# Attention to FFN in one kernel: order of the first mix, the last unit's output and the first transposes

## The reference, cut to what matters

```python
# attention, per batch b and head h (4 x 8), 576 tokens, 64 wide; w_phi: 64 x 128
def phi(x):
    proj = einsum('bhsd,df->bhsf', x, w_phi)
    proj = proj - max(abs(proj), axis=-1)
    return concatenate([exp(proj), exp(-proj)], axis=-1)
q_p, k_p = phi(q), phi(k)
kv = einsum('bhsf,bhsd->bhfd', k_p, v);  z = sum(k_p, axis=2)
x = einsum('bhsf,bhfd->bhsd', q_p, kv) / (einsum('bhsf,bhf->bhs', q_p, z) + 1e-6)
# mix over the tokens and FFN; x is now (4, 576, 512); U: 576 x 32, V: 32 x 576
u = x + transpose(transpose(x) @ U @ V)
x2 = u + relu(u @ w_ch1) @ w_ch2          # w_ch1: 512 x 2048, w_ch2: 2048 x 512
# then a mixture of 8 experts with a held choice (not touched by the change)
```

## Time and profile before

| | before |
|---|---|
| median of three runs | 935.76 us (933.89 to 935.84) |
| the profiled execution | 933.35 us, of which the span of its instructions 931.5 |
| PE busy | 898.2 us, 96% of the span |
| DVE, ACT, POOL busy | 324.1, 250.2, 147.2 us |
| mean granted clock of PE | 0.984 |

### The profile page before, as it was taken

The page is one execution under the profiler, slowest core; times in us unless marked ns, Lnnn a source line. Parts: engine busy times, 40 slices in busy tenths (PEclk is TensorE's granted clock), DMA queues, the critical chain, the costliest instruction groups (busy, mean ns, idle before and its releaser), DMA issues.

```text
span 931.5 us, 18920 instructions
## 1 busy us (share of the span) xinstructions
PE 898.2 (96%) x7112; PEld 788.9 (85%) x7113; DVE 324.1 (35%) x612; ACT 250.2 (27%) x497; POOL 147.2 (16%) x150
## 2 busy tenths in 40 slices
PE   5999999889999999999999999999999999999996
PEld 5999999679999999889988999999877777787774
DVE  4566676421221112122123323211565252332221
ACT  3566766411111111011101111111225342332221
POOL 0211122329000000000000000034332221122111
PEclk9999999979999999999999999999999999999998
DMA  5544442103000000000000000022118151311111
GB/s 130 122 129 108 124 124 73 59 24 114 1 18 18 1 0 35 0 1 34 1 1 1 35 1 12 35 93 88 46 46 304 42 217 39 116 58 34 39 34 40
DMA packets 41884, 55.84 MB, mean 60 GB/s; under 512 B 24944, under 2 KB 25072, under 8 KB 41840
## 3 DMA queue, kind: packets, MB, share of 16 engines
q1 hardware_dynamic: 38320, 44.66, 15.6%
q0 software_dynamic: 3360, 10.49, 3.5%
q10 hardware_dynamic: 160, 0.07, 0.0%
HBM read 45.76 MB, written 9.96 MB: 60 GB/s over the span
## 4 chain that ended last, share of the span: by engine, by line
PE 90%; DVE 3%; issue 3%; ACT 1%; DMA 1%; SPq 0%; ACTq 0%; DVEq 0%; POOL 0%; POOLq 0%
PE bank L1415 22%; PE bank L1417 21%; PE bank L1416 21%; PE bank L1347 7%; PE bank L1363 4%; PE bank L1320 4%; PE bank L1460 2%; PE bank L1588 2%; PE bank L1331 2%; PE bank L1478 2%; PE bank L1483 1%; PE bank L1308 1%; PE bank L1540 1%; DMA rows<-in_moe_w 1%; ACT W L831 1%
## 5 line engine op out<-in xcount | busy, mean ns | idle before, releaser
L957 DVE SCALAR_TENSOR_TENSOR hid_lo<-bank,hid_hi 128x384 fp32r<-128x384 f32 x96 | 53.6, 558 | 320.7 <-ACT hid_hi L806 320.7
L806 ACT ACTIVATE hid_hi<-bank 128x384 fp32r<-128x384 f32 x96 | 47.2, 492 | 375.8 <-PE bank L1417 375.8
L1415 PE MATMUL bank<-uT_hi,W 128*128 128x384 f32 x384 | 130.9, 341 | 1.2 <-DVE uT_lo L974 1.2
L1417 PE MATMUL bank<-uT_hi,W 128*128 128x384 f32 x384 | 130.7, 340 | 0.0
L1416 PE MATMUL bank<-uT_lo,W 128*128 128x384 f32 x384 | 130.2, 339 | 0.0
L1415 PE MATMUL bank<-W,hid_hi 128*128 128x512 f32 x288 | 117.3, 407 | 0.0
L1417 PE MATMUL bank<-W,hid_lo 128*128 128x512 f32 x288 | 115.1, 400 | 0.0
L1416 PE MATMUL bank<-W,hid_hi 128*128 128x512 f32 x288 | 114.3, 397 | 0.0
L1347 PE MATMUL bank<-vv,kp 64*128 64x65 f32 x1152 | 78.2, 284 | 3.0 <-DVE rows L931 3.0
L1415 PEld LDWEIGHTS bank<-uT_hi,W 128*128 128x128 f32 x384 | 73.5, 192 | 5.4 <-DVE uT_lo L974 1.5
L1347 PEld LDWEIGHTS bank<-vv,kp 64*128 64x128 f32 x1152 | 75.3, 202 | 3.2 <-issue 3.2
(11 more groups left out here) (229 smaller groups left out, 1305.4 us busy)
## 6 DMA issues: line engine op xcount, KB each, us to landing
rows<-in_moe_w SPq DMA_DIRECT2D x16, 1024.0 KB, 6.6
stage<-in_moe_w_ch SPq DMA_DIRECT2D x16, 512.0 KB, 4.1
qk_raw<-in_q SPq DMA_DIRECT2D x32, 144.0 KB, 2.9
qk_raw<-in_k SPq DMA_DIRECT2D x32, 144.0 KB, 3.0
vv<-in_v SPq DMA_DIRECT2D x32, 144.0 KB, 3.1
x_rows<-rows SPq DMA_DIRECT2D x6, 768.0 KB
out<-stage,oid_now POOLq DMA_INDIRECT x20, 2.8
u_pair<-in_moe_U SPq DMA_DIRECT2D x4, 72.0 KB, 4.4
```

The costliest lines, as they stand in the source:

```text
L806: act.activation(hid_hi[:, n % 2], bank[:, HB[n % 2], 0:TOK], ACT.Relu).then_inc(hid_hi_out, 1)
L957: dve.scalar_tensor_tensor(out=hid_lo[:, n % 2], in0=bank[:, HB[n % 2], 0:TOK], scalar=0.0, in1=hid_hi[:, n % 2].bitcast(F32), op0=ALU.max ...
L1415: pe.matmul(dst, lhs_hi, rhs_hi, start=start, stop=False)
L1417: return pe.matmul(dst, lhs_lo, rhs_hi, start=False, stop=stop)
```

## The change

On DVE, the first jobs stand behind steps 16 and 17 (so behind the division of unit 14), and the division of unit 15 behind the uT jobs (`first_done`). On ACT, z_hi stands in step 17 behind `exp_k`. On PE, z stays behind step 16, and the three mixes go into step 17, between `turn_q(2)` and `output(0)`. The four uT jobs of the first block take banks 2, 3, 0 and 1 and do not wait for each other; `hidden(0, 0)` waits for one part of uT before each three matmuls; the wait for the last division (`n_out`) goes from `hidden` to `output(0, 0)`; POOL waits for the last output matmuls (`n_done`) and not for the division. The two small buffers of the division leave the overlay, since they are now used while POOL writes there.

```diff
+        den = sb("den", [P, OT[0]])
+        rden = sb("rden", [P, OT[0]])
         attn = ExitStack()
...
-        den = sb("den", [P, OT[0]])
-        rden = sb("rden", [P, OT[0]])
...
-        def attention_steps(eng, step, between=lambda s: None):
+        def attention_steps(eng, step):
...
-            for s in range(UNITS, UNITS + 3):
+            for s in range(UNITS, UNITS + 2):
                 step(s, s % 2, range(s - 2, UNITS))
-                between(s)
...
+        def side_bank(job, n):
+            if job[0] == "uT" and job[1] == 0:
+                return bank[:, (2, 3, 0, 1)[job[2]]]
+            return bank[:, SIDE[n % 2]]
+
+        def is_step(s, n):
+            return isinstance(s, int) and s == n
+
+        def ffn_order(hidden, output, side, early=lambda stage: None, first_done=lambda: None):
             n = EARLY
             for job in first_jobs[EARLY:]:
                 side(job, n)
                 n += 1
+            first_done()
             hidden(0, 0)
...
-            pool.wait_ge(n_out, OUTS * UNITS)
+            pool.wait_ge(n_done, OUTS * UNITS)
...
                 if older:
                     exp_k(s - 2, par, 2)
+                    if is_step(s, UNITS + 1):
+                        side(first_jobs[0], 0)
                     exp_q(0)
...
-                for s in range(UNITS, UNITS + 3):
+                for s in range(UNITS, UNITS + 2):
                     step(s, s % 2, range(s - 3, UNITS))
-                    early_jobs(side)(s)
+                for n in range(EARLY):
+                    side(first_jobs[n], n)
...
-            ffn_order(hidden, output, side, early)
+            ffn_order(hidden, output, side, early, lambda: step(UNITS + 2, UNITS % 2, range(UNITS - 1, UNITS)))
...
                     turn_q(2)
+                    if is_step(s, UNITS + 1):
+                        for n in range(1, EARLY):
+                            side(first_jobs[n], n)
                     output(0)
                     output(1)
+                if is_step(s, UNITS):
+                    side(first_jobs[0], 0)
...
-                if f == 0:
+                if f == 0 and b > 0:
                     pe.wait_ge(side_out, jobs_before["uT", b, KC - 1])
                 if n >= 2:
                     pe.wait_ge(hid_out, n - 1)
-                else:
-                    pe.wait_ge(n_out, OUTS * UNITS)
                 for c in range(KC):
+                    if n == 0:
+                        pe.wait_ge(side_out, jobs_before["uT", 0, c])
...
                 pe.wait_ge(hid_out, n + 1)
+                if n == 0:
+                    pe.wait_ge(n_out, OUTS * UNITS)
...
-                dst = bank[:, SIDE[n % 2]]
-                if n >= 2:
+                dst = side_bank(job, n)
+                if n >= 2 and not (kind == "uT" and b == 0):
                     pe.wait_ge(side_out, n - 1)
```

More of the change, by code:

```diff
@@ L810, in side @@
                     act.wait_ge(side_done, n + 1)
-                    act.activation(z_hi[:, :], bank[:, SIDE[n % 2], 0:DM], ACT.Copy).then_inc(side_hi, 1)
+                    act.activation(z_hi[:, :], side_bank(job, n)[:, 0:DM], ACT.Copy).then_inc(side_hi, 1)
                 elif job[0] == "uT":
                     act.wait_ge(side_done, n + 1)
-                    act.activation(uT_hi[:, job[2]], bank[:, SIDE[n % 2], 0:TOK], ACT.Copy).then_inc(side_hi, 1)
+                    act.activation(uT_hi[:, job[2]], side_bank(job, n)[:, 0:TOK], ACT.Copy).then_inc(side_hi, 1)
             def exp_shifted(j):
@@ L823, in early @@
                     exp_shifted(0)
-            attention_steps(act, step, early_jobs(side))
+            attention_steps(act, step)
             ffn_order(hidden, lambda b, f: None, side, early)
@@ L962, in side @@
                 kind, b, i = job
-                src = bank[:, SIDE[n % 2]]
+                src = side_bank(job, n)
                 dve.wait_ge(side_done, n + 1)
@@ L1522, in early @@
                     mm.then_inc(r_pe, 1)
-            attention_steps(pe, step, early_jobs(side))
+            attention_steps(pe, step)
             pe.wait_ge(gates_loaded, 16 + 16 * KC)
```

## The result

The changed kernel takes 919.13 us (median of four, 917.52 to 922.33) against 934.83 before in the same comparison; the ratio is 0.9849 with a 95% interval of 0.9827 to 0.9871, so by the ratio 14.1 us faster (12.1 to 16.2); the two medians themselves lie 15.7 apart. Run again beside other kernels it took 920.35 (919.00 to 921.84, five runs) against 933.96, ratio 0.9854 (0.9838 to 0.9871), 13.6 us. Forecast were 921.4 and 13.3 saved. The profiled execution took 920.65, its span 918.8 (931.5 before).

The account below looks back on a forecast made before the run. TensorE, with 90% of the chain of waits, was taken to bound the kernel. Savings of 2.99 + 4.52 + 1.60 + 2.66 + 1.55 = 13.3 us from a mean of 934.7 gave 921.4; range 917.6 to 926.0.

Parts of the forecast that it names:

- Steps 1 and 2: Behind z: idle wait for unit 14's division shrinks, 2.99 us saved; unit 15 then runs at high clock, 4.52 saved.
- part 1: Behind z: unit 14's division ahead of z_lo, key exponentials ahead of z_hi; 3.34 us becomes 0.35, 2.99 saved.
- Step 3: Three mixes between turn_q(2) and unit 15's output: 3.45 us becomes 1.85, 1.60 saved.
- Step 4: uT jobs ahead of the first hidden chunk, four banks and waits by chunk: 4.42 us becomes 1.76, 2.66 saved.
- Step 5: First hidden chunk at clock 1.00: 3.63 us becomes 2.08, 1.55 saved; called the least sure term.
- Step 6: Before output(0,0): unit 15's division behind uT_lo, hidden by 0.4 us; second weights' split ready 2.2 before needed.
- Step 7: den and rden moved out of the overlay: taken as 0 us, bound 0.3 either way.
- B: Clock falls over the twelve uT transposes, so the first hidden chunk runs low; 11.6 us saved, 923.1; chance 0.15.
- C: Clock falls already in unit 15's step, which has no projections beside the state; 9.1 us saved, 925.6; chance 0.09.
- D: Unit 15 doesn't start earlier, since something else released its state; at most 5.8 us saved, 929; chance 0.04.
- E: Slower: PE stays at low clock from z's end into the first FFN rounds; 936.6 us and more; chance 0.015.

Follow-up runs that it names:

- e1: Kernel before, with only unit 14's division put ahead of z_lo and the key exponentials ahead of z_hi; 924.03 us, ratio 0.9884 to before.
- e2: Changed kernel with z_lo again ahead of unit 14's division and z_hi ahead of the key exponentials; 927.89 us, ratio 0.9952 to before.
- e8: Changed kernel with the logits matmuls spread among output matmuls and a bank of its own for the third mix; 915.16 us, ratio 0.9797 to before.
- e4: Changed kernel with uT back in two banks, all uT_lo awaited and unit 15's division ahead of them; 922.79 us, ratio 0.9863 to before.
- e9: Second single profile of e4's kernel, nothing else changed; 17.39 us from z's end to output(0,0).
- e10: Second single profile of e1's kernel, nothing else changed; 930.6 us, of it 21.34 from z's end to output(0,0).
- e3: Changed kernel with the three mixes behind unit 15's output again; 921.96 us, ratio 0.9866 to before.
- e5: Changed kernel with each of the first block's twelve uT transposes done four times; 924.15 us, ratio 0.9887 to before.
- e11: Second single profile of the kernel before, unchanged; 27.68 us from z's end to output(0,0).

## Why the prediction was right

Step by step, saved in the forecast and as the two profiles show it:

| step | forecast | measured |
|---|---|---|
| 1 division of unit 14 ahead of z_lo | 2.99 | 3.01 (3.34 to 0.33) |
| 2 unit 15 at the high clock | 4.52 | 4.62 (11.27 to 4.40 + 2.25) |
| 3 mixes between turn and output | 1.60 | 1.28 (3.45 to 2.17) |
| 4 uT in four banks | 2.66 | 2.70 (4.42 to 1.72) |
| 5 first hidden chunk | 1.55 | 1.43 (3.63 to 2.20) |
| sum | 13.3 | 13.04 |

**Steps 1 and 2** were right in size and in cause: e1 does part 1 alone and gains both, e2 takes it away and loses both. The price of the idle stretch was for the greater part the clock behind it. **Step 3** was mis-sized by 0.3: I counted a mix as two starts 0.23 apart, but the third mix's first matmul, behind its wait, takes 0.50 in the chain (189.25), and this is 0.27 of the miss. In e8, where that mix doesn't wait, its first matmul takes 0.23. **Step 4** was right, chain and pace both; e4 gives it 2.24, less than 2.70, because the mixes stand earlier there: before, the first uT_lo came 1.01 behind its uT_hi (201.53 to 202.54), held up by the division of unit 15; in e4 it comes 0.60 behind. **Step 5**, called the least sure, came true in size but for 0.12 (the first hidden matmul comes behind a wait too and takes 0.45 in the chain, the others 0.17), but its reason was incomplete, and that the term came out is in part luck. I put it down to the uT jobs' wait. e4 and e9 keep that wait and the clock stays 1.00, so there the other parts had already saved it. Part 1 alone had not: in e1 and e10 the chunk runs low. In e3 (parts 1 and 4) and in e2 (parts 3 and 4) it runs at 1.00. So the 1.43 us belong to no single part: any two of the three gave them in these profiles. **Step 6** held with 0.67 us to spare for the output (0.4 forecast) and 2.26 for the split. **Step 7** (the buffers' addresses) was not tried by itself; the parts of both traces behind output(0,0), with three falls behind logits each, take 720.4 and 720.6 us, which leaves little for it. The chances of the forecast add up to 1.01, a slip that changes nothing.

Of the rivals, B fell by e5, C and D by e1. E, the slower side, would have needed some 30 us of low clock; the longest low stretch between z and output(0,0) was 13.7 (e2), and in the changed kernel there was none. By the ratios the kernel gained 14.1 and 13.6 us, by the profiles 13.04 locally; the rest is within the scatter by executions that I had set at 2 to 3 us. That a part of this scatter is the clock behind the logits is likely from the differing falls of the two profiles of one kernel, but was not measured by itself.

## What to carry to other kernels

Where PE bounds a kernel and idles for some microseconds at a hand-over, read the granted clock behind the idle time as well: here 3 us of idle time cost 7 to 8.6. Look in the queue of the engine that PE waits for: short operations that were ready (the division on DVE, the keys' exponentials on ACT) stood behind ones that waited for 8 us of matmuls, and reordering the two queues was worth more than half of the whole change. Put small dependent pieces where dense work covers their round trip, and break up groups of tiny matmuls among dense ones.

## What the runs showed of the hardware that I had not expected

**Work that holds the high clock was slow to bring it back.** Unit 14's state runs at 1.00; the same instructions for unit 15, entered at 0.50, stayed there for 8.55 us in e2 with PE busy all the time, and the low stretch ended only in the output behind the mixes. In the kernel before it lasted 10.2 us and ended in the mixes. In e11 it lasted 6.8 and ended within the output's own matmuls (the row at 193.23, at 0.69), so this work can bring the clock back, only later and not at a fixed time. Behind the logits, where dense matmuls follow, a low stretch took 3.41 us in nearly every case (6.8 once, in e10).

**A group of tiny matmuls can bring the clock down without any idle time.** 24 matmuls of 9 columns in 2.6 us, PE busy throughout, are followed by 3.41 us at 0.50 behind two to three of the FFN's five groups, and not always the same ones (in all eleven profiles that have them whole); spread over 4 us among dense ones they are not, in both kernels that have them so (ten groups). What decides which groups are followed by a fall stays open.

**The clock column is silent before its first record.** In the profile of the kernel before it reads 1.00 from 12 to 30 us:

```profile
12.00:30.00 18.00, 15.55 (x162) 15.13 (x160) 8.16 (x9) 7.04 (x16) 0.00 (x0) 1.00 0.18 51
```

In the changed kernel's it reads 0.50 in the same part of the attention:

```profile
19.00:32.00 13.00, 13.00 (x154) 12.88 (x152) 3.83 (x4) 4.85 (x12) 0.00 (x0) 0.50 0.19 43
```

But in the chain of the kernel before 24 state matmuls take 2.45 us at 20.38, and 1.29 us at 35.23 once a record exists; in the changed one they take 2.46 at 19.72 and 1.29 at 35.53. So both ran low there. The mean clock of a span (0.984 in both) therefore does not compare the two kernels; durations of like instructions do.
